# Seven block products for eight in the up multiplications of two feed-forward layers

## The reference

```
g   = x @ w_gate                 # 2304x512 by 512x1536
val = x @ w_val                  # the same shape
x1  = (silu(g) * val) @ w_out    # 1536 -> 512
h   = x1 @ w_in                  # 512 -> 2048
a   = h if h >= 1, 0 if h <= -1, (h + 1)**2 / 4 between
out = a @ w_out2                 # 2048 -> 512
```

## Time and profile before

| | |
|---|---|
| median of three runs | 1120.67 us |
| the profiled execution, its own time | 1118.66 us |
| its span, first to last instruction | 1116.5 us |
| TensorE busy | 1074.3 us (96%), 7376 matmuls |
| VectorE, ScalarE, GpSimd busy | 490.6, 457.6, 156.3 us |
| mean granted TensorE clock | 0.992 of full |

### The profile page before, as it was taken

How to read it: one execution, slowest core, us unless ns; L and a number is a source line. 1 busy time by engine, 2 the same in 40 slices (tenths; PEclk the granted TensorE clock), 3 DMA queues, 4 the chain that set the end, 5 groups by cost and what they waited for, 6 DMA issues and landing times.

```text
span 1116.5 us, 21580 instructions
## 1 busy us (share of the span) xinstructions
PE 1074.3 (96%) x7376; PEld 969.4 (87%) x7376; DVE 490.6 (44%) x1258; ACT 457.6 (41%) x1070; POOL 156.3 (14%) x196
## 2 busy tenths in 40 slices
PE   4989898999999999999999999999999999999997
PEld 2656566669999999999999999999999999999996
DVE  4777777764322212121212123565435344444443
ACT  3666666665322212121212122564434344444433
POOL 4555555535200000000000000000000000000000
PEclk9899999999999999999999999999999999999999
DMA  5233233225200000000000001230000000000000
GB/s 184 59 93 92 92 92 92 79 69 171 95 1 1 0 0 0 0 0 0 0 0 0 0 1 58 73 135 1 29 1 29 0 28 0 0 28 0 29 1 28
DMA packets 35285, 43.50 MB, mean 39 GB/s; under 512 B 9904, under 2 KB 20144, under 8 KB 35248
## 3 DMA queue, kind: packets, MB, share of 16 engines
q1 hardware_dynamic: 35248, 43.02, 12.2%
HBM read 38.29 MB, written 4.72 MB: 39 GB/s over the span
## 4 chain that ended last, share of the span: by engine, by line
PE 89%; issue 4%; DVE 3%; ACT 2%; DMA 1%; DVEq 1%; POOL 0%; SPq 0%; ACTq 0%; POOLq 0%
PE ps L993 20%; PE ps L995 19%; PE ps L994 19%; PE ps L1064 6%; PE ps L1065 6%; PE ps L1063 6%; PE ps L969 4%; PE ps L940 4%; PE ps L921 4%; ACT rown L515 1%; PE ps L962 1%; DMA zb<-z 1%; DVE xy L750 1%; DVE den L730 1%; DVE pt L741 0%
## 5 line engine op out<-in xcount | busy, mean ns | idle before, releaser
L993 PE MATMUL ps<-xh,w 128*128 128x288 f32 x768 | 227.3, 296 | 1.1 <-issue 1.1
L994 PE MATMUL ps<-xl,w 128*128 128x288 f32 x768 | 226.7, 295 | 0.0
L995 PE MATMUL ps<-xh,w 128*128 128x288 f32 x768 | 225.8, 294 | 0.0
L830 DVE TENSOR_TENSOR hid<-hid,ps 128x288 f32<-128x288 f32 x96 | 43.6, 454 | 249.3 <-ACT hid L599 249.3
L993 PEld LDWEIGHTS ps<-xh,w 128*128 128x128 f32 x768 | 143.9, 187 | 1.3 <-issue 1.3
L995 PEld LDWEIGHTS ps<-xh,w 128*128 128x128 f32 x768 | 144.6, 188 | 0.0
L994 PEld LDWEIGHTS ps<-xl,w 128*128 128x128 f32 x768 | 144.2, 188 | 0.0
L599 ACT ACTIVATE hid<-ps 128x288 f32<-128x288 f32 x96 | 39.3, 410 | 254.7 <-PE ps L995 254.7
L995 PE MATMUL ps<-yh,w 128*128 128x384 f32 x384 | 129.5, 337 | 0.0
L993 PE MATMUL ps<-yh,w 128*128 128x384 f32 x384 | 129.3, 337 | 0.0
L994 PE MATMUL ps<-yl,w 128*128 128x384 f32 x384 | 129.0, 336 | 0.0
(11 more groups left out here) (75 smaller groups left out, 1745.7 us busy)
## 6 DMA issues: line engine op xcount, KB each, us to landing
raw<-w_out SPq DMA_DIRECT2D x28, 256.0 KB, 2.9
qk<-qT SPq DMA_DIRECT2D x16, 288.0 KB, 2.9
qk<-kT SPq DMA_DIRECT2D x16, 288.0 KB, 3.2
out<-out_sb SPq DMA_DIRECT2D x6, 768.0 KB, 3.5
qn<-q_rest SPq DMA_DIRECT2D x16, 256.0 KB, 2.9
vm<-v_rest SPq DMA_DIRECT2D x16, 256.0 KB, 3.2
raw<-w_in SPq DMA_DIRECT2D x16, 256.0 KB, 2.6
raw<-w_gate SPq DMA_DIRECT2D x12, 256.0 KB, 2.6
```

Of the source, the lines that this page charges most:

```text
L993: nc.tensor.matmul(dst, w_hi, v_hi, start=start, stop=False)
L994: nc.tensor.matmul(dst, w_hi, v_lo, start=False, stop=False)
L995: return nc.tensor.matmul(dst, w_lo, v_hi, start=False, stop=stop)
```

## The change

Both layers now go over three superblocks of 768 tokens, in two halves of 384 (`HALF`). An up step takes two hidden tiles at once (layer 1: the gate tile and the val tile; layer 2: two tiles) against the two halves of the tokens and the two halves of the 512 features: a product of 2 x 2 by 2 x 2 blocks. `product` makes it from seven block products of 2 x 3 matmuls, after Winograd's form of Strassen's method, instead of eight. For it the weights need four sums and differences (`up_sums`, slots 4 to 7, GpSimd, 256 columns each) and x four (`x_diff` on VectorE, `x_sums` on GpSimd, 768 columns each). Seven weight operands and seven x operands are split into high and low parts (`up_high`, `up_low`, `x_high`, `x_low`), the weights anew in every step, x once per superblock. The output blocks are P1 + P2 (c11), U2 + P6 (c12), P5 + U3 (c22) and c21 in PSUM; `copy_p1`, `copy_p5` and `copy_u2` bring products to SBUF, since a later product adds onto the same bank. Layer 1 has 36 steps, layer 2 has 24.

The down part is done in units of one 128-feature chunk, one half of the tokens and a group of two hidden tiles: 2 x 3 matmuls of 384 columns, in alternating banks 6 and 7, and VectorE adds each unit onto `xy` (`add_down`, or copies for the first group). Units run two groups behind the up steps and stand between the products: four a step in layer 1, eight in layer 2. In layer 2 they use the weights as the stationary operand. Weights are no longer kept: 512 KB of up weights is loaded per step, 512 KB of down weights per group, and split again for every superblock. The activation of layer 2 is a Relu on ScalarE and two instructions on VectorE (`s_half`, `g_half`). The output leaves transposed, from `xy`, and is turned on the host. There are no loops in the feed-forward part of the program any more. For the first superblock the parts of x are made in attention's last iteration.

The diff, cut to its core (the waits of `silu`, `prod` and the like, and the old functions that go, are left out; the vector engine's steps at the superblocks' borders, where `ends` marks a superblock's last step and `fresh` its first, are shown for layer 1):

```diff
+        PRODUCTS = ((1, 0, True), (4, 2, True), (2, 1, True), (5, 0, False), (6, 2, False), (7, 0, False),
+                    (3, 0, False))
+        PIECES = ((1, 4), (4, 6), (6, 8))
...
+        def unit_range(u):
+            if u < STEPS1:
+                a = UNITS // 2 * u - UNITS * LAG
+                return range(max(a, 0), max(a + UNITS // 2, 0))
+            a = UNITS * (GROUPS1 + u - STEPS1 - LAG)
+            return range(a, a + UNITS)
...
+            def load_up(u):
+                if u == 2:
+                    sp.wait_ge(x_done, len(PARTS) * NPAIR)
+                at_least(sp, up, 7 * (u - 2))
+                sp.dma_start(wu_r[u % 3][:, 0:4], w_up[u % S1 if u < STEPS1 else S1 + (u - STEPS1) % S2]
+                             .rearrange("p (k n) -> p k n", k=4)).then_inc(ld_up[u % 3], 16)
...
+            for u in range(STEPS):
+                if u < STEPS1 and u % 2 == 0:
+                    load_down(u // 2)
+                if u >= STEPS1:
+                    load_down(GROUPS1 + u - STEPS1)
+                if u + 2 < STEPS:
+                    load_up(u + 2)
+                if u > STEPS1 + S2 and (u - STEPS1) % S2 == LAG + 1:
+                    sb = (u - STEPS1) // S2 - 1
+                    at_least(sp, evac, UNITS * (GROUPS1 + NF2 // 2 * (sb + 1)))
+                    cols = slice(SB * sb, SB * sb + SB)
+                    sp.dma_start(out.rearrange("(c p) n -> p c n", p=P)[:, :, cols], xy[:, :, cols]).then_inc(stored, 16)
...
+            def up_sums(u):
+                w = wu_r[u % 3]
+                at_least(pool, ld_up[u % 3], 16 * (u // 3 + 1))
+                nc.gpsimd.tensor_tensor(w[:, 4], w[:, 0], w[:, 3], ALU.add).then_inc(sums, 1)
+                pool.wait_ge(sums, 4 * u + 1)
+                nc.gpsimd.tensor_tensor(w[:, 5], w[:, 4], w[:, 1], ALU.subtract).then_inc(sums, 1)
+                pool.wait_ge(sums, 4 * u + 2)
+                nc.gpsimd.tensor_tensor(w[:, 6], w[:, 2], w[:, 5], ALU.subtract).then_inc(sums, 1)
+                nc.gpsimd.tensor_tensor(w[:, 7], w[:, 1], w[:, 0], ALU.subtract).then_inc(sums, 1)
+            def up_low(u):
+                a, b = PIECES[0]
+                pool.wait_ge(sums, 4 * u + 4)
+                pool.wait_ge(wu_hi[0], u + 1)
+                nc.gpsimd.tensor_tensor(wu_l[u % 3][:, a:b], wu_r[u % 3][:, a:b], wu_h[u % 2][:, a - 1:b - 1].bitcast(F32),
+                                        ALU.subtract).then_inc(wu_lo[0], 1)
...
+            def down_low(t):
+                pool.wait_ge(wd_hi, t + 1)
+                nc.gpsimd.tensor_tensor(wd_l[:, t % 6], wd_r[:, t % 6], wd_h[:, t % 6].bitcast(F32),
+                                        ALU.subtract).then_inc(wd_lo, 1)
...
+            for u in range(STEPS):
+                if u + 1 < STEPS:
+                    up_low(u + 1)
+                for t in down_tiles(u):
+                    down_low(t)
+                if u + 2 < STEPS:
+                    up_sums(u + 2)
+                if u + 1 < STEPS and superblock(u + 1) != superblock(u):
+                    x_sums(superblock(u + 1), 0)
+                    x_sums(superblock(u + 1), 1)
...
+                if u > 0:
+                    hid_high(u - 1)
+                copy_p1(u)
+                if fresh:
+                    x_high(sb, 4)
+                copy_p5(u)
+                if fresh:
+                    x_high(sb, 5)
+                if ends:
+                    x_high(sb + 1, 0)
+                up_high(u + 1, 1)
+                up_high(u + 1, 0)
+                for t in down_tiles(u):
+                    down_high(t)
+                up_high(u + 1, 2)
+                if fresh:
+                    x_high(sb, 6)
+                if ends:
+                    x_high(sb + 1, 1)
+                copy_u2(u)
+                if ends:
+                    x_high(sb + 1, 2)
+                silu(u)
+                if ends:
+                    x_high(sb + 1, 3)
...
+                    hid_high(tiles_of(u)[0] - 1)
+                if more:
+                    up_high(u + 1, 1)
+                copy_p5(u)
+                if fresh:
+                    x_high(sb, 5)
+                if ends:
+                    x_high(sb + 1, 0)
+                if more:
+                    up_high(u + 1, 0)
+                    up_high(u + 1, 2)
+                if fresh:
+                    x_high(sb, 6)
+                copy_u2(u)
+                if ends:
+                    x_high(sb + 1, 1)
+                for t in down_tiles(u):
+                    down_high(t)
+                if ends:
+                    x_high(sb + 1, 2)
+                relu_half(u, 0)
+                if ends:
+                    x_high(sb + 1, 3)
+                copy_c21(u)
+                relu_half(u, 1)
+                hid_high(tiles_of(u)[0])
+            hid_high(2 * NGROUP - 1)
...
+            def up_low(u, n):
+                a, b = PIECES[n]
+                dve.wait_ge(sums, 4 * u + 2 + n)
+                dve.wait_ge(wu_hi[n], u + 1)
+                nc.vector.tensor_tensor(wu_l[u % 3][:, a:b], wu_r[u % 3][:, a:b], wu_h[u % 2][:, a - 1:b - 1].bitcast(F32),
+                                        ALU.subtract).then_inc(wu_lo[n], 1)
...
+            def x_low(sb, n):
+                dve.wait_ge(x_hi, 7 * sb + n + 1)
+                if n in (1, 3):
+                    dve.wait_ge(tp, 2 * sb + (1 if n == 1 else 2))
+                src = {0: x_quarter(0, sb, 0), 2: x_quarter(1, sb, 0), 4: x_quarter(1, sb, 1)}
+                nc.vector.tensor_tensor(xt_l[:, n], src[n] if n in src else xt_r[:, n],
+                                        xt_h[:, n].bitcast(F32), ALU.subtract).then_inc(x_lo, 1)
...
+            def c11(u):
+                at_least(dve, p1_c, u + 1)
+                at_least(dve, up, 7 * u + 3)
+                if u < STEPS1:
+                    at_least(dve, prod_done, 2 * (u - 1))
+                else:
+                    at_least(dve, prod_done, 2 * min(u - 1, STEPS1))
+                    at_least(dve, g_done, 2 * (u - STEPS1) - 2)
+                nc.vector.tensor_tensor(hb[:, u % 2, 0, 0:HALF], p1s[:], ps[:, bank_of(u, 2), 0:HALF],
+                                        ALU.add).then_inc(c11_d, 1)
+            def c12(u):
+                at_least(dve, u2_c, u + 1)
+                at_least(dve, up, 7 * u + 5)
+                nc.vector.tensor_tensor(hb[:, u % 2, 0, HALF:], u2s[:], ps[:, bank_of(u, 4), 0:HALF],
+                                        ALU.add).then_inc(c12_d, 1)
+            def c22(u):
+                at_least(dve, p5_c, u + 1)
+                at_least(dve, up, 7 * u + 6)
+                nc.vector.tensor_tensor(hb[:, u % 2, 1, HALF:], p5s[:], ps[:, bank_of(u, 5), 0:HALF],
+                                        ALU.add).then_inc(c22_d, 1)
...
+            def add_down(n):
+                g, c, t = n // UNITS, n % UNITS // 2, n % 2
+                at_least(dve, dn, n + 1)
+                y, o = x_half(c, group_block(g), t), ps[:, 6 + n % 2, 0:HALF]
+                if first_group(g):
+                    nc.vector.tensor_copy(y, o).then_inc(evac, 1)
+                else:
+                    at_least(dve, evac, n + 1 - UNITS)
+                    nc.vector.tensor_tensor(y, y, o, ALU.add).then_inc(evac, 1)
...
+            for u in range(STEPS1):
+                sb = superblock(u)
+                fresh = u > 0 and superblock(u - 1) != sb
+                ends = superblock(u + 1) != sb
+                units = list(unit_range(u))
+                if u > 0:
+                    hid_low(u - 1)
+                if fresh:
+                    x_low(sb, 3)
+                if ends:
+                    x_diff(sb + 1, 0)
+                if fresh:
+                    x_low(sb, 4)
+                c11(u)
+                for n in units[0:1]:
+                    add_down(n)
+                if fresh:
+                    x_low(sb, 5)
+                if ends:
+                    x_low(sb + 1, 0)
+                up_low(u + 1, 1)
+                c12(u)
+                for n in units[1:2]:
+                    add_down(n)
+                up_low(u + 1, 2)
+                if fresh:
+                    x_low(sb, 6)
+                if ends:
+                    x_low(sb + 1, 1)
+                c22(u)
+                for n in units[2:3]:
+                    add_down(n)
+                prod(u, 1)
+                if ends:
+                    x_diff(sb + 1, 1)
+                prod(u, 0)
+                if ends:
+                    x_low(sb + 1, 2)
+                for n in units[3:4]:
+                    add_down(n)
+            for u in range(STEPS1, STEPS):
+                sb = superblock(u)
+                fresh = superblock(u - 1) != sb
+                more = u + 1 < STEPS
...
+            def product(u, n):
+                slot, bank, fresh = PRODUCTS[n]
+                sb = superblock(u)
+                pe.wait_ge(wu_lo[piece_of(slot)], u + 1)
```

(54 more changed lines are left out.)

641 lines of the change are left out of this document (290 added, 351 removed).

## The result

The changed kernel takes **1140.11 us** median (1137.61 to 1141.32, 4 runs), the kernel before 1121.21 (1119.37 to 3623.67, 4 runs; the long one took three times as long as the others for a reason that no trace shows, and is left out of the ratio). The ratio is 1.0171, 95% interval [1.0145, 1.0198]: slower by 1.7%. The interval lies clear of 1, though the difference is under the two per cent that the prediction gave as what a measurement here can tell. Forecast were 1108 us and 1070 to 1136, so the prediction was wrong, in its value, its range and its sign. The profiled execution took 1140.93 us, its span is 1139.0.

What follows compares the result with a forecast made beforehand. TensorE, by its feed-forward matmuls, was the bound. 1118.7 - 64.7 (matmuls) + 8 (steady) + 5 (start) + 32 (borders) + 2 (clock) + 3 (attention) + 2 (tail) = 1106, plus 2 for the median: 1108 us, range 1070 to 1136.

Steps and rivals of the forecast that it cites:

- Matmuls: Feed-forward layers: 4536 matmuls of 384 columns, 0.176 us apart, 798.3 us in all, a gain of 64.7 us.
- Rival 4: Feed-forward layers: the product count does not fall as said; excluded by the lists of matmuls, no chance given.
- Rival 3: Feed-forward layers: matmuls 0.17 us apart instead of 0.176, 27 us less, 1081 us; chance 0.08.
- First four steps: Start of the feed-forward part: no down units to fill waits, 1.2 us a step, 5 us (3 to 8).
- Steady steps: Layer 1: seventh product waits 0.25 us for c22 in 31 steps, 8 us (0 to 22); layer 2: 0.
- Mutual exclusion: VectorE's instructions with two SBUF tiles and GpSimd's exclude each other; 8.3 of 11.62 us in layer 1, 13.4 of 15.84 in layer 2.
- Borders: Five changes of superblock: preparing x makes VectorE and GpSimd late, 6.5 us each, 32 us (20 to 45).
- The clock: TensorE's granted clock falls after a wait of c22 at a border: 2 us (0 to 10).
- Attention: Last iteration of attention: preparing the first superblock's x fits but adds to chains, 3 us (0 to 7).
- Tail: Kernel's end: last group of two waits for VectorE, +3, shorter output store, -1; together +2 us (1 to 4).
- Rival 1: Whole kernel: TensorE stays the bound everywhere, the engines' order absorbs the waits; 1077 us, chance 0.20.
- Rival 2: Every step: up_low 2 and c22 late, 1.5 us a layer 1 step, 0.8 in layer 2; 1172 us, chance 0.12.

Runs made afterwards that it cites:

- experiment 7: The kernel of experiment 6 without GpSimd's four sums of up weights, 1 MB loaded per step, output not the reference's: 1092.17 us.
- Experiments 1 and 2: Two separate runs: experiment 1, and the changed kernel with GpSimd's x_sums 0 moved ahead of the down weights' low part and the four sums at borders, 1119.63 us.
- experiment 1: The changed kernel with own memory for raw x operands 1 and 3 from superblock 1 on: 1121.18 us.
- experiment 8: The changed kernel without the preparation of x at the five borders, output not the reference's: 1077.78 us.
- experiment 4: The changed kernel with GpSimd's sums for the first two steps moved into attention's first iteration: 1130.83 us.
- experiment 6: The kernel of experiment 5 with VectorE reordered: x_low later at attention's end, g_half and additions before the two hid_low at the kernel's end: 1105.48 us.
- experiment 5: The changed kernel with the edits of Experiments 1 and 2 and experiment 4 together: 1115.73 us.
- x1_behind_c22: The changed kernel with x_low 1 behind c22 on VectorE at borders, in layer 2 also behind additions 3 and 4: 1128.09 us.

## Why the prediction was wrong

- **Matmuls: the count right, the distance a little too long.** 4536 of them, but 0.1737 us apart and not 0.176: 15.63 us for a step of 90 in layer 2, and 11.47 for one of 66 in layer 1 where nothing waits (experiment 7). The term of 798.3 us is 10.4 too high. Rival 4 is out. Rival 3's 0.17 isn't reached, but 10 of its 27 us are there.
- **First four steps, right:** 5.5 for 5. The loads cost nothing, as said; 512 KB land in 4.4 us:

```profile
wu_r<-w_up SPq DMA_DIRECT2D x60, 512.0 KB, 4.4
```

- **Steady steps, right:** the seventh product waits for c22 in every step of layer 1, and the step is 0.26 us longer than its 66 matmuls (11.73 for 11.47), where I had 0.25. The prediction counted 31 such steps where there are 27, so its 8 us were 7. The table's -0.4 is these 7 less what the shorter distance gives back in 3402 matmuls, 8 us; that the table shows next to nothing there is luck, a real wait and a shorter distance that cancel. Layer 2 waits for nothing, as said.
- **Mutual exclusion, right:** VectorE's low parts of 512 columns average 1238 ns where I had 690 alone, GpSimd's of 768 columns 1977 where I had 1830. The product with a PSUM operand is untouched, the one with two SBUF inputs is not:

```profile
L943 DVE TENSOR_TENSOR wu_l<-wu_r,wu_h 128x512 fp32r<-128x512 f32 x120 | 148.6, 1238 | 6.0 <-POOL wu_r L547 5.7 <-ACT wu_h L676 0.3
L1026 DVE TENSOR_TENSOR hid_r<-hb 128x384 f32<-128x384 f32 x36 | 26.4, 733 | 1.3 <-ACT hb L728 1.0
L1026 DVE TENSOR_TENSOR hid_r<-hb,ps 128x384 f32<-128x384 f32 x36 | 19.9, 553 | 10.4 <-PE ps L1244 10.4
```

  The Trainium skill ("SBUF — State Buffer", section "Who interferes with whom") says that a VectorE instruction with two SBUF inputs contends with a GpSimd instruction that reads SBUF, and that one with at most one SBUF input, outside the two-port modes, does not. These rows agree: 733 ns with two SBUF inputs, 553 with one.
- **Borders, the step that failed most:** 6.5 us each and 32 in all, measured 61.6. The sum of the work was not the main mistake: with the wait cured 43 to 46 us are left, 6 to 10 of them the clock's, so 35 to 39 of waits against my 32, inside the bounds of 20 to 45. With all x preparation gone it is 0. What was missing is a wait of 4.7 us in layer 1 and 6.3 in layer 2: I costed x_low by its engine's time and never asked what it waits for, though the tp wait stands in its code. Experiments 1 and 2 show that it is worth 15 to 17 us of the 61.6, with the clock behind it. That the remaining 3 to 7 us come from instructions that the walks took at their durations alone, and that take 2 us and more beside GpSimd, is my reading; no run tells them apart.
- **The clock, failed:** 2 us forecast, 10.9 at the borders and 2.6 in the last step. I had put the wait's length beside one row and charged it once in five. At each border some 15 matmuls run at the lower level. They come with the waits: there are none at the borders of experiment 8, where TensorE has no wait. But a wait's length doesn't settle it. In experiment 1 TensorE is idle for the same 2.24 us in steps 11, 23 and 35; the clock stayed at 1.00 in the first and the third and fell in the second, for 10 matmuls.
- **Attention, the second step that failed:** 3 us forecast, 16.8 measured. The part behind the first iteration, where the change puts four sums of GpSimd ahead of ScalarE's and VectorE's pieces, has no term in my sum, though the prediction's own rows show TensorE waiting there before the change: it lost 7.0 us, and experiment 4 gives 8.2 back. The last iteration has a term, 3 us for chains, from durations against idle time. Its 1701st to 1800th matmuls lost 7.0, because x_low 1 waits for x_sums 0 here too and holds the maxima; experiment 6 gives 4.2 back. The matmuls just ahead lost 1.1 and the last ones gained 1.5, as forecast in kind. The 2.9 us between, from matmul 268 to 1600, are within what that stretch varies between executions.
- **Tail, right in its mechanism:** the walk has the first addition of the last but one group, behind both hid_low, end 5.1 us after the last step where TensorE wants its bank at 2.1. It comes out so: TensorE stands idle 2.8 us (its next start is 2.95 late), and this is gone in experiment 6. The other 2.6 of the 5.8 us are the clock's, behind this wait.
- **The rivals.** Rival 1's 1077 us and the 1077.78 of the kernel without x at its borders agree by chance: rival 1 has 10 us at the borders and 3 in attention, that kernel 0 and 17. Rival 2 had the wrong place: c22 costs 0.26 in steady steps of layer 1, not 1.5. The slower side was reached by two waits of which no rival spoke, x_low 1 for x_sums 0 and the first step's pieces for late sums, and by the clock.

Added up on the profiled execution: 1106 + 13.8 (attention) + 27.6 (borders and clock) - 8.4 (steady steps and distance) + 2.8 (last step) + 0.5 (start) is 1142.3. Behind the last matmul's start come 3.7 us where there were 6.1, which is 1.5 less than forecast: 1140.8, where 1140.93 was measured.

## What to carry to other kernels

Before an instruction is costed, read every wait ahead of it, those for shared memory too: an instruction that needs no result of another engine can still stand behind that engine's whole queue, and all that is behind it in its own. For each new wait follow the releasing engine's queue up to the instruction that releases, and do it at the rare places (first iteration, borders, tail) as for the steady step; here the steady steps were right and the rare places cost 84 us (borders 61.6, attention 16.8, last step 5.8). To tell a stage's loss from its spread between executions, compare the times between the same instructions by their number, place by place: attention varies by 10 us as a whole, mostly between the two places that were changed, which vary by 3 and less. When two cures of a place don't add up, as in experiment 5, they cured the same wait; what was left here was for the most part VectorE's own work, which at layer 2's borders fills the two steps.

## What the runs showed of the hardware that was not expected

Equal waits at equal places did not bring equal clocks. In experiment 1 the wait of 2.24 us before the seventh product ends at 540.72 in step 23 and at 692.78 in step 35. TensorE is as busy in the window around each, 2.77 of 5 us, and the granted clock fell only in the first:

```profile
538.00:543.00 5.00, 2.77 (x11) 2.48 (x10) 5.00 (x6) 0.41 (x1) 4.84 (x6) 0.79 0.00 0
690.00:695.00 5.00, 2.77 (x17) 2.48 (x16) 5.00 (x7) 0.48 (x1) 4.84 (x6) 1.00 0.00 0
```

The same holds for the wait of 2.95 us before the last step's third unit, which seven profiles have: 17 or 18 matmuls ran at the lower level behind it in two of them, 11 in four, and one in x1_behind_c22. With it the last step's excess is 3.1 to 5.8 us. So a forecast can give a wait of 2 to 3 us a range for the clock, 0 to 2.6 us here, and no single value. In attention has 0.50 after only 2.01 us. Behind the 6.5 us of step 11 it stood at 0.50 for the next 5 us.

TensorE's distance at 384 columns is 0.1737 us in long unbroken stretches, below the 0.176 of a stretch of twelve.
